# Loading q and k with three neighbouring tokens on a partition, and turning them head by head

## What is computed

```
# attention: B=4, H=8, S=768, D=64; chunks of 32 queries, 16 keys to the left, 8 to the right, 8 memory keys
for c in range(nc):
    q_c = q[:, :, c_start:c_end]
    k_full = concatenate([mem_k, k[:, :, l_start:r_end]]); v_full likewise
    scores = scale * q_c @ k_full^T;  a = softmax(scores)
    out[:, :, c_start:c_end] = a @ v_full
x = out as (B*S, H*D) = (3072, 512)
# first MLP: h = x @ w_in (512 -> 2048); g = P(h) / Q(h), a rational function; x = g @ w_out
# second MLP: out = ((x @ w1) * (x @ w2) @ w3) @ w_out2
```

## Time and profile before

| | us |
|---|---|
| median of 3 runs (1126.63 to 1129.42) | 1127.97 |
| the profiled execution | 1123.61 |
| its span | 1121.8 |

### The profile page before, as it was taken

The page is one execution under the profiler, slowest core; times in us unless marked ns, Lnnn a source line. Parts: engine busy times, 40 slices in busy tenths (PEclk is TensorE's granted clock), DMA queues, the critical chain, the costliest instruction groups (busy, mean ns, idle before and its releaser), DMA issues.

```text
span 1121.8 us, 16430 instructions
## 1 busy us (share of the span) xinstructions
PE 1083.9 (97%) x6292; PEld 892.7 (80%) x6292; DVE 706.5 (63%) x995; ACT 581.9 (52%) x960; POOL 169.7 (15%) x137
## 2 busy tenths in 40 slices
PE   7998796799999999999999999999999999999998
PEld 6877675688888888888888888888888888888886
DVE  5378776899999999999998998811212121111211
ACT  3457664677866876877787787521213122121311
POOL 4324543512122122121100100100000000000000
PEclk9999988899999999999999999999999999999999
DMA  9989996211211220121100145320202010020000
GB/s 297 268 221 245 248 251 159 76 57 47 85 56 47 72 68 29 55 86 45 56 37 0 37 150 220 118 75 1 76 0 75 0 37 37 0 75 0 37 1 38
DMA packets 138734, 97.66 MB, mean 87 GB/s; under 512 B 89548, under 2 KB 118220, under 8 KB 137676
## 3 DMA queue, kind: packets, MB, share of 16 engines
q1 hardware_dynamic: 138700, 97.21, 28.6%
HBM read 65.74 MB, written 31.46 MB: 87 GB/s over the span
## 4 chain that ended last, share of the span: by engine, by line
PE 51%; DVE 25%; issue 4%; ACT 2%; ACTq 0%; DVEq 0%
PE banks L1198 23%; PE banks L1213 11%; PE banks L1182 9%; PE banks L205 8%; DVE nr L1101 5%; DVE nr L1098 5%; DVE nr L1105 4%; DVE g_lo L1110 3%; DVE sq L1081 3%; DVE poly L1088 3%; DVE poly L1091 1%; DVE x_lo L1067 1%; ACT y_sb L1003 1%; ACT sq L980 0%; ACT poly L981 0%
## 5 line engine op out<-in xcount | busy, mean ns | idle before, releaser
L1182 PE MATMUL banks<-g_hi,weights 128*128 128x512 f32 x768 | 253.9, 392 | 5.5 <-DVE g_lo L1110 5.5
L205 PE MATMUL banks<-x_hi,weights 128*128 128x512 f32 x768 | 251.5, 390 | 1.9 <-PEq L215 1.9
L1198 PE MATMUL banks<-x_hi,weights 128*128 128x512 f32 x768 | 244.2, 389 | 0.0
L1139 DVE TENSOR_TENSOR nr<-habs,banks 128x512 f32<-128x512 f32 x48 | 33.0, 688 | 256.7 <-ACT habs L1033 256.7
L1182 PEld LDWEIGHTS banks<-g_hi,weights 128*128 128x128 f32 x768 | 145.3, 189 | 38.2 <-DVE g_lo L1110 7.5
L205 PEld LDWEIGHTS banks<-x_hi,weights 128*128 128x128 f32 x768 | 144.4, 188 | 32.0 <-issue 2.0
L1198 PEld LDWEIGHTS banks<-x_hi,weights 128*128 128x128 f32 x768 | 144.1, 188 | 29.8
L1033 ACT ACTIVATE habs<-banks 128x512 f32<-128x512 f32 x48 | 28.6, 596 | 245.2 <-PE banks L1198 245.2
L1182 PE MATMUL banks<-g_lo,weights 128*128 128x512 f32 x384 | 150.4, 392 | 0.0
L205 PE MATMUL banks<-x_lo,weights 128*128 128x512 f32 x384 | 149.5, 389 | 0.0
L1198 PE MATMUL banks<-x_lo,weights 128*128 128x512 f32 x384 | 149.4, 389 | 0.0
(11 more groups left out here) (83 smaller groups left out, 1539.7 us busy)
## 6 DMA issues: line engine op xcount, KB each, us to landing
x_raw<-x_transposed_dram SPq DMA_DIRECT2D x12, 1024.0 KB, 5.2
weights<-second_mlp_weights_dram SPq DMA_DIRECT2D x8, 1536.0 KB, 6.3
second_mlp_weights_dram<-split SPq DMA_DIRECT2D x16, 512.0 KB, 3.0
v_sb<-in_v SPq DMA_DIRECT2D x44, 160.0 KB
qk_sb<-in_q SPq DMA_DIRECT2D x24, 256.0 KB, 4.1
x_transposed_dram<-xt_sb SPq DMA_DIRECT2D x24, 256.0 KB, 2.8
x_transposed_dram<-y_sb SPq DMA_DIRECT2D x6, 1024.0 KB, 4.9
out<-y_sb SPq DMA_DIRECT2D x5, 1024.0 KB, 4.2
```

Source lines behind the costliest of these rows:

```text
L205: last = nc.tensor.matmul(bank[m % 4][:, :], slot[:, m, a, cols], x[:, c, :], start=c == 0 and n == 0, stop=c == KC - 1 and n == 2)
L1182: last = nc.tensor.matmul(bank[4 + c][:, :], slot[:, m, a, cols], g[:, m % G_BUFS, :], start=m == 0 and n == 0, stop=m == SLOTS - 1 and n ...
L1198: last = nc.tensor.matmul(bank[2 * (j % 2) + w][:, :], bslot[:, j, 2 + 2 * w + a, cols], x[:, c, :], start=c == 0 and n == 0, stop=c == KC ...
```

## The change

q and k are loaded by a half batch at once: 384 tokens as 128 partitions with three neighbouring tokens each. Three tokens of a head are neighbours in memory, so a run is 192 values or 768 bytes. k no longer has its neighbours of the other half in this load; they come in one small load of 8 or 16 tokens (`load_edge`) into 32 rows that are set to zero at the start. A half batch has three loads in place of seven: 24 in all in place of 56.

A partition now holds tokens 3p, 3p+1 and 3p+2, and the three tokens of one head lie side by side, so a pair of heads is no longer 128 neighbouring values. A turn therefore takes one head and one of the three tokens at a time: 6 ordinary products of 64 columns of weights (the data) with the 128 columns of the identity, which write 64 partitions of the bank at every third column (a step of 12 bytes). A turn of k has one more transpose for the edge rows, which writes columns 0 to 15 and 400 to 415.

```
-Q_ROWS, Q_AT = (128, 128, 128), (0, 128, 256)
-K_ROWS, K_AT = (96, 96, 96, 120), (0, 96, 192, 288)
-QK_TURNS = ((2, 3), (4, 5, 6), (0, 1))
+RUN = HALF // P
+EDGE = LEFT
+Q_LOAD, K_LOAD, EDGE_LOAD = range(3)
+QK_TURNS = ((K_LOAD, EDGE_LOAD), (), (Q_LOAD,))
...
+def edges(ap):
+
+    return bass.AP(ap.tensor, ap.offset, [list(ap.ap[0]), [HALF + EDGE, 2], [1, EDGE]])
...
+            def load_q(hb):
+
                 b, f = hb // 2, hb % 2
+                sp.dma_start(qk_sb[:, f, 0, 0:RUN * DM].rearrange("p (h c) -> p h c", h=H),
+                             q[b, :, f * HALF:(f + 1) * HALF, :].rearrange("h (p e) d -> p h (e d)", e=RUN))\
+                    .then_inc(q_loaded[f], 16)
+
+            def load_k(hb):
...
+            def load_edge(hb):
+
+                b, f = hb // 2, hb % 2
+                row, at, n = ((EDGE, HALF, RIGHT), (0, HALF - LEFT, LEFT))[f]
+                sp.dma_start(qk_sb[row:row + n, f, 1, RUN * DM:(RUN + 1) * DM].rearrange("p (h d) -> p h d", h=H),
+                             k[b, :, at:at + n, :].rearrange("h s d -> s h d")).then_inc(k_loaded[f], 16)
+
+            def load_qk(hb, loads):
+
+                for n in loads:
+                    if hb >= 2:
+                        sp.wait_ge(turned, 1 + TURNED * (hb - 2) + (PAIRS if n == Q_LOAD else TURNED))
+                    (load_q, load_k, load_edge)[n](hb)
...
                 if i == 0:
-                    load_qk(0, range(Q_GROUPS + 1, QK_GROUPS))
+                    load_qk(0, (EDGE_LOAD,))
                 if i == 1:
-                    load_qk(1, range(0, 2))
+                    load_qk(1, (Q_LOAD,))
...
-            nc.vector.memset(qk_sb[0:LEFT, 0, 1, 0:DM], 0.0).then_inc(k_zeroed, 1)
-            nc.vector.memset(qk_sb[P // 2:P, 1, 1, (K_GROUPS - 1) * DM:K_GROUPS * DM], 0.0).then_inc(k_zeroed, 1)
+            nc.vector.memset(qk_sb[0:2 * EDGE, :, 1, RUN * DM:(RUN + 1) * DM], 0.0).then_inc(k_zeroed, 1)
...
             def turn(b, f, c):
 
                 w, a = c // PAIRS, c % PAIRS
-                at, rows = ((Q_AT, Q_ROWS), (K_AT, K_ROWS))[w]
-                pe.wait_ge((q_loaded, k_loaded)[w][f], 16 * len(rows) * (b + 1))
+                at = (0, EDGE)[w]
+                pe.wait_ge((q_loaded, k_loaded)[w][f], 16 * (w + 1) * (b + 1))
                 pe.wait_ge(turned_copied, 1 + TURNED * (2 * b + f) + c)
-                for g, n in enumerate(rows):
-                    last = nc.tensor.transpose(bank[7][:, at[g]:at[g] + n],
-                                               qk_sb[0:n, f, w, g * DM + a * P:g * DM + (a + 1) * P], ident[0:n, 0:n])
+                heads = qk_sb[:, f, w, 0:RUN * DM].rearrange("p (h e d) -> p h e d", h=H, e=RUN)
+                for e in range(RUN):
+                    for h in range(2):
+                        rows = slice(D * h, D * (h + 1))
+                        last = nc.tensor.matmul(bank[7][rows, at:at + HALF].rearrange("p (t e) -> p e t", e=RUN)[:, e, :],
+                                                heads[:, 2 * a + h, e, :], ident[:, :], start=True, stop=True)
+                if w == 1:
+                    last = nc.tensor.transpose(edges(bank[7]), qk_sb[0:2 * EDGE, f, 1, RUN * DM + a * P:RUN * DM + (a + 1) * P],
+                                               ident[0:2 * EDGE, 0:2 * EDGE])
                 last.then_inc(turned, 1)
```

More of the change, by code:

```diff
@@ L51 @@
 SPAN = LEFT + HALF + RIGHT
-Q_ROWS, Q_AT = (128, 128, 128), (0, 128, 256)
-K_ROWS, K_AT = (96, 96, 96, 120), (0, 96, 192, 288)
-Q_GROUPS, K_GROUPS = len(Q_ROWS), len(K_ROWS)
-QK_GROUPS = Q_GROUPS + K_GROUPS
-QK_TURNS = ((2, 3), (4, 5, 6), (0, 1))
+RUN = HALF // P
+EDGE = LEFT
+Q_LOAD, K_LOAD, EDGE_LOAD = range(3)
+QK_TURNS = ((K_LOAD, EDGE_LOAD), (), (Q_LOAD,))
 TURNED = 2 * PAIRS
@@ L293, in _ @@
         def _(sp):
-            def load_q(hb, g):
+            def load_q(hb):
                 b, f = hb // 2, hb % 2
[L296 to L300, removed]
+                sp.dma_start(qk_sb[:, f, 0, 0:RUN * DM].rearrange("p (h c) -> p h c", h=H),
+                             q[b, :, f * HALF:(f + 1) * HALF, :].rearrange("h (p e) d -> p h (e d)", e=RUN))\
+                    .then_inc(q_loaded[f], 16)
@@ L301, in load_k @@
+            def load_k(hb):
                 b, f = hb // 2, hb % 2
[L302 to L317, removed]
+                sp.dma_start(qk_sb[:, f, 1, 0:RUN * DM].rearrange("p (h c) -> p h c", h=H),
+                             k[b, :, f * HALF:(f + 1) * HALF, :].rearrange("h (p e) d -> p h (e d)", e=RUN))\
+                    .then_inc(k_loaded[f], 16)
@@ L365, in _ @@
                              mem_k[b, :, :, :].rearrange("h s d -> s h d")).then_inc(memk_loaded, 16)
-            sp.wait_ge(k_zeroed, 2)
-            load_qk(0, range(0, Q_GROUPS + 1))
+            sp.wait_ge(k_zeroed, 1)
+            load_qk(0, (Q_LOAD, K_LOAD))
             for i in range(JS):
@@ L377, in _ @@
                 if i == 0:
-                    load_qk(0, range(Q_GROUPS + 1, QK_GROUPS))
+                    load_qk(0, (EDGE_LOAD,))
                 if i == 1:
-                    load_qk(1, range(0, 2))
+                    load_qk(1, (Q_LOAD,))
                 if i == 2:
-                    load_qk(1, range(2, 4))
+                    load_qk(1, (K_LOAD,))
                 if i == 3:
-                    load_qk(1, range(4, QK_GROUPS))
+                    load_qk(1, (EDGE_LOAD,))
                     sp.wait_ge(v_zeroed, 1)
@@ L393, in _ @@
                 if i == 5:
-                    load_qk(2, range(0, Q_GROUPS))
+                    load_qk(2, (Q_LOAD,))
                 if i == 6:
-                    load_qk(2, range(Q_GROUPS, QK_GROUPS))
-            load_qk(3, range(0, 2))
+                    load_qk(2, (K_LOAD, EDGE_LOAD))
+            load_qk(3, (Q_LOAD,))
             def tile_step(t):
```

## The result

| | before | changed |
|---|---|---|
| median of 4 runs, us | 1127.93 (1126.63 to 1129.42) | 1140.18 (1139.22 to 1141.56) |
| profiled execution, us | 1123.61 | 1139.22 |
| its span, us | 1121.8 | 1137.4 |

The ratio is 1.0112 (95% interval 1.0098 to 1.0127): the change costs 12.25 us, where 15 were predicted.

The account below looks back on a forecast made before the run. PE was taken to bound the fold stage and early tiles, DMA the later tiles, then PE all. Fold stage +10.3, tiles +9.1, last batch -4.4 gave +15 us: 1143 from 1127.97, range 1129 to 1155 (main case 1135 to 1152).

Parts of the forecast that it names:

- The bound: First block: PE limits the fold stage and tiles 0 to 6, DMA later tiles; changed, PE limits all 18, DMA share under 0.9.
- The price of a turn: On PE in the fold stage, a turn of q goes from 0.33 to 0.92 us, one of k from 0.41 to 1.11.
- rival (b): Turns on PE stream one cycle a column and cost no more than before; loads bring 16 us, 1112 us; chance 0.08.
- (c): Writing every third column of the bank halves the rate, 0.66 us more per turn, 1185 us; chance 0.07.
- The price of a change of shape: On PE, between groups of different array shape: 0.13 us per change with the refill, bounds 0 and 0.15.
- Rival (a): Shape changes on PE cost nothing more; a turn's mean extra is 0.32 us, +2.5 us, 1130.5 us; chance 0.15.
- The fold stage: Before tile 0: 16 new turns between products of full shape, +0.59 us per q and +0.70 per k, +10.3 us.
- The tiles: Tiles 0 to 17: PE's pace goes from 4.44 to 5.69 us and sets the time, 102.4 against 93.3, +9.1 us.
- The last batch: From tile 18 on: with DMA and SP relieved, tile 20 follows tile 19 by 6.0 us, not 10.4; -4.4 us.
- The shift of the median: Whole kernel: +15 us, summed on the profiled 1123.6 us, applies unchanged to the median of 1127.97, giving 1143.
- The loads by themselves: In the tiles, new loads save 0.67 us of DMA time per tile, taking the DMA's pace from 5.65 to 4.98 us.
- The price of a packet: On one DMA engine, 18.2 ns for 256 bytes and 38.9 for 768, the latter interpolated between 512 bytes and 2 KB.

Follow-up runs that it names:

- experiment 4: The changed kernel with each product of a turn writing 128 neighbouring columns of the bank, not every third: 1140.30 us, ratio 1.0119 to the kernel before.
- Experiment 3: The changed kernel with a turn's six products reordered, three of one head and then three of the other: 1155.98 us, ratio 1.0256 to the kernel before.
- experiment 5: The changed kernel with the edge transpose made as two ordinary products in the turn's own shape: 1137.03 us, ratio 1.0093 to the kernel before.
- experiment 2: The kernel before, old loads kept, each transpose of a head pair split into two ordinary products of one head: 1138.56 us, ratio 1.0114.
- experiment 1: The changed kernel's loads with full-width transposes for turns (wrong columns, old amount of work, plus edge transposes): 1119.36 us, ratio 0.9941 to the kernel before.
- experiment 6: The kernel before with the new load and turn for q alone, only from half batch 2 on: 1125.65 us, ratio 0.9980.
- experiment 7: As experiment 6, but q's turns stand after scores and after pv, k's old transposes first: 1125.75 us, ratio 0.9995 to the kernel before.
- experiment 8: As experiment 7, with all loads of k issued in the step of a half batch's first tile: 1123.10 us, ratio 0.9969 to the kernel before.

## Why the prediction was right, and where its sizes were off

**The bound.** Right. PE is full in the fold stage and in all 18 tiles, the waits for the store are gone, and the DMA share is 0.85 (under 0.9 was forecast). 1140.18 lies 2.8 us under the forecast. Some of the nearness is luck: the fold stage came out 0.7 us above its term, the tiles 2.0 below, the last batch 0.6 above, and these misses cancel in part.

**The price of a turn.** Right. A turn of q was put at 0.92 us and one of k at 1.11. The fold stage shows 1.01 and 1.18, of which 0.08 are in the product behind and were paid there before as well (0.31 in place of 0.23); that leaves 0.93 and 1.10. Against rival (b), one cycle a column, stands the turn itself (0.71 us between starts where it has no change of shape on the way out) and the 0.11 us from pair to pair; against (c) experiment 4. Experiment 3 showed the overlap of the halves, but the pairs are not as strict as the working had them.

**The price of a change of shape.** Right in kind, near in size. The working took 0.13 us with the refill, that is, until the next group runs at its pace. In the fold stage the turn of q has 0.93 - 0.66 = 0.27 us beside its stream, 0.13 for each of two changes. The starts alone show 0.09 on the way in and 0.09 on the way out (0.80 against 0.71), `pv` is 0.15 us shorter behind a turn of q and 0.10 behind an edge, and experiment 5 takes off 0.10 us a change by nothing but the shape. Rival (a), no cost, would have put tile 0 near 76 us (70.70 + 16 x 0.32); it began at 83, or 82 without the late start.

**The fold stage.** +10.3 forecast, +11.0 measured after the later start is taken off. The new turns cost what was put; the old ones, which they replace, were put at the 0.33 and 0.41 us of a tile, and took 0.26 and 0.29 here (0.34 and 0.37 less the same 0.08). That is 1.1 us more for the 12 turns that do stand between fold products. The working had all 16 there, but two turns of q and one of k stand behind scores, whose shape isn't the full one either, and the last stands ahead of tile 0; these four cost 2.1 us where 2.6 were put.

**The tiles.** +9.1 forecast, +7.1 measured. The term that was mis-sized is what the turns give back beside `pv`. By kind of tile the working gives +1.12, +1.47 and +1.14 (three turns of q; one of q and two of k; two of k); measured against the first three tiles of before, 4.43, 4.61 and 4.27, it is +1.03, +1.35 and +1.04. Each tile came out 0.1 us cheaper. It can be placed in the second turn. The timeline of PE before, tile 0, from its second turn on:

```profile
73.19 0.55 PE L711 MATMUL banks<-ident,qk_sb 128*128 128x128 f32 x3
73.67 1.15 PE L752 MATMUL banks<-pT,v_sb 96*64 96x64 f32 x32
74.75 0.55 PE L711 MATMUL banks<-ident,qk_sb 128*128 128x128 f32 x3
```

Second turn and `pv` took 0.48 + 1.08 = 1.56 us; in the changed kernel's tile 3 they take 0.71 + 0.93 = 1.64, +0.08. The working had +0.33 for the stream less one change of 0.13, +0.20. More than one change's worth came back where turn and `pv` share a shape. Turns of k show the same at that place, +0.37 and +0.33 (tiles 1 and 2) where +0.44 was put. So PE's pace is 5.58 and not 5.69, which makes 2.0 us over 18 tiles.

**The last batch.** -4.4 forecast, -3.8 measured. Tile 20 begins 6.6 us after tile 19 where 6.0 were put and 10.4 stood. With the old loads experiment 2 has 8.8, and its last batch takes 33.6 us in place of 35.1; with the new loads alone it takes 32.5 (experiment 1). So the loads bring 2.3 to 2.6 of the 3.8, and slower tiles ahead of the last batch the rest.

**The shift of the median.** The sum was made against one execution and carried to the median unchanged. The stages of the two profiled executions give 15.6 us, near the 15; the medians give 12.25. The rest is that before's profiled execution was a fast one by 4.3 us, and after's by 1.0. A start that is 1.4 us later by no work of the change is of the same kind; without it the stages give 14.2.

**The loads by themselves.** The price of a packet was right: in the records of the first 200 us the mean is 18.1 ns for 256 bytes and 38.9 for 768. The pace of the DMA engines was not. The working read 5.65 us a tile from tiles 7 to 17 alone. Share times length over all 18 tiles gives 1.01 x 93.3 / 18 = 5.2 us of DMA work a tile before, 5.3 in experiment 2, and 4.7 with the new loads both in the changed kernel (0.85) and in experiment 1 (0.98). So the loads save about 0.5 us a tile and not 0.67, from a lower start. The forecast didn't suffer, since PE's pace lies above either; what was expected of experiments 1 and 2 did. Rival (b) let the loads bring 16 us if the turns cost nothing. Experiment 1 brings 7.8, with the DMA engines full at 4.79 us a tile and PE, with the edge transposes, at 4.60 close beneath.

**Sums.** Three of the working's don't come out as written, and no reading hangs on them. Rival (a) by the formula 64 D - 17.8 is +2.7 and not +2.5. The upper bound of what the loads save, with 27.7 ns a packet, is 1.15 us a tile and not 1.3. And 94 changes of shape (40 in the fold stage, 54 in the tiles) at 0.08 to 0.15, with the last batch at its bounds, give 1137 to 1149 and not 1135 to 1152.

What stays open: whether a layout with 768-byte packets could be turned without splitting a pair of heads. With three tokens of one head side by side the two heads of a pair are 192 values apart, and no other turn of it was tried; nor was a way to leave the edge transpose out.

## What to carry to other kernels

Longer packets are worth only what the engine behind them leaves: before trading DMA time for PE time, write down both paces per tile (here 4.7 us of DMA work, by share and length, against 5.58 on PE) and take the larger. Between products of two tiling shapes count about 0.1 us on each side, so keep a group's shape that of its neighbours; a small product in a shape of its own costs more by its shape than by its columns. The halves of this change did not add up, so run each half alone.

## What the runs showed of the hardware

- A change of shape on PE costs about 0.1 us (experiment 5, six changes and 0.59 us less in three tiles), or 0.13 with the refill (the turn of q in the fold stage). The Trainium skill ("TensorEngine Tiling (Array Packing)", Key Properties) says that changing the tiling mode drains the engine; the trace agrees and puts this number to it.
- A write to every third float32 of a bank streams as fast as a contiguous one (0.80 and 0.81 us a turn).
- Products in the two column halves overlap even where the program does not alternate them: 1.07 us a turn where a strict sequence would be 1.3 and alternation is 0.80.
- In experiment 6 a wait of 2.19 us on PE, in a stretch of 4 us in which it was busy for 1.81, was followed by 8 us at a granted clock of 0.50, the level of 1.2 GHz; the tile took 9.0 us in place of 4.23. In experiment 7 the wait of 3.35 us was followed by 4 us at a mean of 0.73, and the tile took 9.9 in place of 4.91. So a wait of PE cost more than itself.
- Packets of 768 bytes took 38.9 ns in the mean of the 16,384 records of the changed kernel, where the line between the rows for 512 bytes and 2 KB gave the same; in experiment 8 they took 41.1.
